# Chunk 0's state behind the turning of its outputs, and another order of tile 0's attention jobs

## What is computed

```python
for t in range(S):
    y[:, :, t] = np.einsum('bhd,bhde->bhe', q[:, :, t], state)
    v_old = np.einsum('bhde,bhd->bhe', state, k_n[:, :, t])
    state = state + beta_t * np.einsum('bhd,bhe->bhde', k_n[:, :, t], v[:, :, t] - v_old)
```

## Time and profile before

| | us |
|---|---|
| median of 3 runs | 997.12 |
| lowest, highest | 996.5, 997.6 |
| the profiled execution's own time | 997.04 |
| its span in the trace | 994.6 |
| PE busy | 953.7 |
| VectorE busy | 734.0 |
| ScalarE busy | 517.8 |
| GpSimd busy | 333.1 |

### The profile page before, as it was taken

How to read it: one execution, slowest core, us unless ns; L and a number is a source line. 1 busy time by engine, 2 the same in 40 slices (tenths; PEclk the granted TensorE clock), 3 DMA queues, 4 the chain that set the end, 5 groups by cost and what they waited for, 6 DMA issues and landing times.

```text
span 994.6 us, 23444 instructions
## 1 busy us (share of the span) xinstructions
PE 953.7 (96%) x9960; PEld 794.5 (80%) x9960; DVE 734.0 (74%) x1132; ACT 517.8 (52%) x854; POOL 333.1 (33%) x417
## 2 busy tenths in 40 slices
PE   3579999999999999999999999999999999999998
PEld 3578878888888888888788888888888888888897
DVE  5977886778687777856746668768778778687775
ACT  5664744563655456444645545545555455554543
POOL 2089748804940791296002793100101001001000
PEclk9669999999999999999999999999999999999999
DMA  9314113102200310111006311000102001010011
GB/s 213 64 36 95 33 51 66 49 17 46 64 9 19 66 49 2 24 29 48 17 4 222 96 32 64 1 1 24 41 1 65 1 11 54 0 31 3 1 33 32
DMA packets 110679, 42.50 MB, mean 43 GB/s; under 512 B 89040, under 2 KB 105936, under 8 KB 110576
## 3 DMA queue, kind: packets, MB, share of 16 engines
q1 hardware_dynamic: 105984, 39.73, 16.1%
q10 hardware_dynamic: 4592, 1.28, 0.7%
HBM read 31.56 MB, written 9.44 MB: 41 GB/s over the span
## 4 chain that ended last, share of the span: by engine, by line
PE 80%; DVE 10%; POOL 5%; issue 2%; ACT 1%; DMA 1%; ACTq 0%; DVEq 0%; POOLq 0%
PE quad L1865 15%; PE bank L1843 8%; PE bank L1844 8%; PE bank L1845 8%; PE quad L1872 8%; PE bank L1865 7%; PE quad L1843 4%; PE quad L1845 4%; PE quad L1844 4%; PE bank L1872 3%; POOL inv L566 3%; DVE blk L1037 2%; POOL blk L563 2%; PE quad L1863 1%; DVE inv L1138 1%
## 5 line engine op out<-in xcount | busy, mean ns | idle before, releaser
L1364 DVE TENSOR_TENSOR g_lo<-tmp,g_hi 128x512 fp32r<-128x512 f32 x192 | 155.4, 810 | 6.6
L1843 PE MATMUL bank<-x_hi,wi_hi 128*128 128x512 f32 x372 | 146.6, 394 | 1.3 <-issue 1.3
L1844 PE MATMUL bank<-x_lo,wi_hi 128*128 128x512 f32 x372 | 145.0, 390 | 0.0
L1845 PE MATMUL bank<-x_hi,wi_lo 128*128 128x512 f32 x372 | 145.0, 390 | 0.0
L1865 PE MATMUL quad<-g_hi,wo_hi 128*128 128x512 f32 x368 | 143.6, 390 | 0.0
L1865 PE MATMUL quad<-g_hi,wo_lo 128*128 128x512 f32 x368 | 143.4, 390 | 0.0
L566 POOL TENSOR_TENSOR inv<-inv,blk 128x31 f32<-128x31 f32 (+15 forms) x155 | 120.2, 776 | 12.1
L1872 PE MATMUL quad<-g_lo,wo_hi 128*128 128x512 f32 x368 | 117.3, 389 | 0.0
L603 POOL TENSOR_TENSOR x_lo<-x_raw,x_hi 128x1536 fp32r<-128x1536 f32 x6 | 23.2, 3859 | 269.2 <-ACT x_hi L635 269.2
L1362 DVE CAST g_hi<-tmp 128x512 fp32r<-128x512 f32 x192 | 98.0, 511 | 20.2 <-PE quad L1872 0.5
L929 ACT ACTIVATE tmp<-bank,consts 128x512 f32<-128x512 f32 x72 | 49.7, 690 | 119.0 <-PE bank L1845 119.0
(11 more groups left out here) (220 smaller groups left out, 1940.5 us busy)
## 6 DMA issues: line engine op xcount, KB each, us to landing
stage<-in_moe_w_in SPq DMA_DIRECT2D x32, 192.0 KB, 3.2
stage<-in_moe_w_out SPq DMA_DIRECT2D x8, 768.0 KB, 5.1
qn<-in_q SPq DMA_DIRECT2D x24, 192.0 KB
x_t<-x_res SPq DMA_DIRECT2D x6, 768.0 KB, 3.4
x_raw<-x_t SPq DMA_DIRECT2D x6, 768.0 KB, 5.0
res_v<-in_v SPq DMA_DIRECT2D x22, 192.0 KB, 3.7
out_x<-res SPq DMA_DIRECT2D x160, 24.0 KB, 1.5
kn<-in_k SPq DMA_DIRECT2D x32, 96.0 KB, 3.1
```

Of the source, the lines that this page charges most:

```text
L1364: nc.vector.tensor_tensor(lo, g, hi.bitcast(FP32), ALU.subtract).then_inc(g_ready, 1)
L1843: mm(dst, wi_hi[:, ft, kt, :], hi[:, kt, :], start=(kt == 0), stop=False)
L1844: mm(dst, wi_hi[:, ft, kt, :], lo[:, kt, :], start=False, stop=False)
L1845: last = mm(dst, wi_lo[:, ft, kt, :], hi[:, kt, :], start=False, stop=(kt == KT - 1))
```

## The change

`first_state()` moves on PE from the first slot of tile 0 to the end of `first()`, right behind `turn_late()` and ahead of product1(0). On VectorE `low_weights(1)` moves behind the two that make the low halves of x. In tile 0, PE's jobs T0 (of chunk 2), M1, F1, V0 and SN0 take other slots, and S0 of chunk 2 goes behind KS1. ScalarE's and VectorE's calls for them move along; on VectorE the turnings and the scaling of the inverse go to slots 11 to 13 from 9 and 11, and the four `take_blocks(2, g)` to slots 21 and 23 from 19, 20 and 21. V0 gets a lent bank and SN0 loses one. No computation is added or removed.

```diff
-ORDER_1 = ("Q0", "KS0", "P0", "T1", "S1", "T0", "M1", "F1", "V0", "SN0", "S0", "KS1", "Y0", "V1", "Q1", "SN1", "P1",
+ORDER_1 = ("Q0", "KS0", "P0", "T1", "S1", "T0", "M1", "F1", "V0", "SN0", "KS1", "S0", "Y0", "V1", "Q1", "SN1", "P1",
...
-LENT_1 = {"KS0": 4}
+LENT_1 = {"KS0": 4, "V0": 18, "KS1": 20, "V1": 22, "SN1": 24, "Y1": 26}
...
@@ ScalarE, attention_1
             take_transposes(2, "T1", knT[:, fill_of(2, 1)])
             yield
             yield
+            take_transposes(2, "T0", knT[:, fill_of(2, 0)])
+            yield
+            yield
             high_weights(5)
             yield
             yield
-            take_transposes(2, "T0", knT[:, fill_of(2, 0)])
             yield
             yield
             fill_diagonal(1, 1)
+            yield
             fill_diagonal(1, 0)
-            yield
-            yield
             yield
             take_outer(1, 0)
...
@@ VectorE, first
             low_weights(0)
-            low_weights(1)
             take_x(0, 0, "YT0")
             take_late_x()
+            low_weights(1)
             low_weights(2)
...
@@ VectorE, attention_1
             take_s(2, 1, "S1")
             yield
+            yield
+            yield
             turn_solved(1)
+            yield
             scale_inverse(1)
             yield
-            yield
             turn_inverse(1)
             yield
-            yield
             take_inner(1, 0)
+            yield
             take_inner(1, 1)
             yield
             yield
-            yield
             take_last_outer(1)
             yield
             take_delta(1, 0, "V0")
             yield
             take_state(1, 0, "SN0")
             yield
+            take_rest(1, 1, "KS1")
             take_s(2, 0, "S0")
+            yield
             take_blocks(2, 0)
             take_blocks(2, 1)
             yield
-            take_rest(1, 1, "KS1")
+            take_delta(1, 1, "V1")
+            yield
             take_blocks(2, 2)
-            yield
             take_blocks(2, 3)
-            yield
-            take_delta(1, 1, "V1")
-            yield
             yield
             take_state(1, 1, "SN1")
...
@@ PE, first and attention_1
             turn_late()
+            first_state()
 
         def attention_1():
 
-            first_state()
             yield
...
             gram(2, 1)
             yield
-            yield
-            yield
             keys_transposed(2, 0)
             yield
+            yield
+            yield
+            yield
+            yield
             merge_inner(1, (0, 1))
             yield
             yield
             yield
-            yield
             merge_outer(1, (0, 1))
             yield
             solve_values(1, 0, "V0")
             yield
             add_to_state(1, 0, "SN0")
+            yield
+            keys_on_state(1, 1, "KS1")
             gram(2, 0)
-            yield
-            yield
-            keys_on_state(1, 1, "KS1")
             yield
             read_out(1, 0, "Y0")
```

More of the change, by code:

```diff
@@ L89 @@
             place_contents(_c, _job)
[L90 to L93, removed]
+            lent = LENT_1 if _c == 1 else LENT
+            if _job in lent:
+                lend(_c, _job, lent[_job])
         elif _c + 1 < NCH:
@@ L1233, in attention_1 @@
             yield
+            take_inner(1, 0)
             yield
-            take_inner(1, 0)
             take_inner(1, 1)
-            yield
             yield
@@ L1249, in attention_1 @@
             yield
-            take_rest(1, 1, "KS1")
-            take_blocks(2, 2)
-            yield
-            take_blocks(2, 3)
-            yield
             take_delta(1, 1, "V1")
             yield
+            take_blocks(2, 2)
+            take_blocks(2, 3)
             yield
@@ L1712, in attention_1 @@
             yield
+            keys_transposed(2, 0)
             yield
             yield
-            keys_transposed(2, 0)
+            yield
+            yield
             yield
             merge_inner(1, (0, 1))
-            yield
             yield
@@ L1726, in attention_1 @@
             add_to_state(1, 0, "SN0")
-            gram(2, 0)
-            yield
             yield
             keys_on_state(1, 1, "KS1")
+            gram(2, 0)
             yield
```

## The result

The changed kernel took 1009.86 us (median of 4 runs, 1008.79 to 1011.59) where the kernel before took 997.36 us beside it: a ratio of 1.0126, 95% interval 1.0108 to 1.0144. It is slower by 12.5 us, and the forecast was 7 us. The profiled execution took 1010.21 us with a span of 1007.8 us; that of before took 997.04 with 994.6, so the two traces differ by 13.2 us, and that is the sum to be explained.

A forecast was written before the change was run, and what follows sets the result against it. The prediction took TensorE as the bound (busy 953.7 of 994.6 us). Lead at step 12, late solve and half clock, -1.0 + 6.3 + 1.7 = 7.0 us on 997.04, gave 1004.0 us (range 1001.0 to 1007.0), chance 0.58.

The forecast's parts named there:

- the front: Start of tile 0: state's matmuls fill PE's idle 1.93 us, clock stays at 2.4 GHz, product 2 of step 0 gains 2.2 us.
- s: How far PE is ahead at product 1 of step 12, tile 0: 2.2 - 1.2 = 1.0 us, bounds -0.3 and 2.9.
- clock falls at the front after all: Rival, start of tile 0: half clock despite the filled gap, product 2 of step 0 at 81.8, total 1005.6 us; chance 0.18.
- stop of 1.33 us: PE's wait near 137 us, no releaser: half kept, 0.7 us goes; if a late instruction block, wholly there again.
- 208.05 - s: Tile 1: forecast start of product 2 of step 21, which started at 201.75 before; 5.3 us later.
- late solve: GpSimd's solve of chunk 2 starts later, behind V1 and main(12), takes 49.1 us; costs 6.3 - s in tile 1.
- about even: Tile 0: new waits behind GpSimd's solve of chunk 1, less waits that go, lose 1.2 us net.
- hidden: Rival, tile 1: solve of chunk 2 takes 43 us or less, so its late start costs nothing; 996.0 us; chance 0.06.
- cancelled: Rival: solve of 46 us, 2.9 us lead and no clock price give 997.3 us, no change; chance 0.04.
- The clock behind the wait: Tile 1, after PE's 6.3 us standstill: matmuls run at half clock for a while, costing 1.7 us.
- no price in tile 1: Rival: full clock is granted soon after PE's wait in tile 1, total 1002.3 us; chance 0.14.
- PE is full, before as after: Behind 208 us: PE has no new waits, later chunks' slack is unchanged, nothing is gained or lost.

The follow-up runs named there:

- after_quiet: Changed kernel, with SyncE's load of weight piece 3 and what it issues after held back until the state's matmuls are done: 1005.25 us, ratio 1.0076.
- rest_only: Changed kernel with its front put back as before, so only the new order of tile 0's jobs is left: 1005.59 us, ratio 1.0078.
- blocks_late: Kernel before, with only the turning of blocks 2 and 3 of chunk 2 moved behind V1 and main(12) on VectorE: 1005.48 us, ratio 1.0078.
- front_split: Kernel before, low_weights(1) behind the low halves of x, half the state's matmuls at the front, half in tile 0's first slot: 997.18 us, ratio 0.9999.
- after_blocks_early: Changed kernel with all four blocks of chunk 2 turned earlier on VectorE, before V1: 1003.34 us, ratio 1.0055.
- after_quiet_early: Changed kernel with the load of weight piece 3 held back and the four blocks of chunk 2 turned earlier: 1000.39 us, ratio 1.0024.
- front_only: Kernel before with the front part of the change alone (state's matmuls and low_weights(1) moved), tile 0's order as before: 1000.49 us, ratio 1.0027.
- front_quiet: Kernel before with the front part of the change and the load of weight piece 3 held back: 997.47 us, ratio 1.0002.

## Why the prediction was wrong in size and right in kind

**The step that failed: the front.** The prediction put the moved state into 1.93 us of idle time and priced it by its own busy time, "2.01 us", so that PE "will have no idle time at all" from 72 to 74.6. The matmuls did start there, behind the turning of y_late. But 29 of 128 came 3.64 us later, the clock fell, and out(0) was 3.3 us late instead of 2.2 early. At in(12), behind which the rest of the sum is set up, the miss is 4.6 us (s = -3.62 for 1.0), and holding the load back gave 4.6 us of the time back (after_quiet). The rival "clock falls at the front after all" had the clock right and still priced out(0) at 81.8, because it too took the state as one unbroken run. The prediction even knew the mechanism: it named the instruction queue as a possible cause of the stop of 1.33 us, and did not ask the same of 128 small instructions moved into 2 us in which the DMA share was 0.86 and then 1.30. At its old place the state did not stop, because the packet was there in time. In the trace of before, 76.2 to 76.3 us:

```profile
q8 instruction: 1, 0.02, 85.9%
```

That packet ends at 77.6, and the state's first matmul came at 80.38.

**The rest of the sum held.** Set up on s, how far TensorE is ahead at in(12), the formula "208.05 - s" for out(21) can be held against four kernels:

| kernel | in(12) | s | 208.05 - s | out(21) measured |
|---|---|---|---|---|
| changed kernel | 148.22 | -3.62 | 211.67 | 211.45 |
| rest_only | 143.42 | 1.18 | 206.87 | 206.64 |
| after_quiet | 143.70 | 0.90 | 207.15 | 206.91 |
| blocks_late | 144.96 | -0.36 | 208.41 | 208.02 |

It is 0.2 to 0.4 us high each time. So the late solve was right in place, mechanism and size. Only s was not: it was forecast 1.0 and came as -3.62.

**Tile 0, "about even": right in size, by luck in part.** The 1.2 us lost from out(0) to in(12) was worked out for a TensorE that comes early. In rest_only, which does, it is 82.39 - 79.96 = 2.43 at out(0) and 1.18 at in(12), 1.25 lost. Its waits were 0.79, 1.56 and 0.28 us where 0.5, 1.65 and 0.4 had been put. But the stop of 1.33 us, of which the prediction kept half, is in none of the five kernels with the new order. The other losses must then have been 0.7 us larger than it put them, and the two errors cancel. In the changed kernel, which comes late to the solve of chunk 1, the loss is 3.62 - 3.31 = 0.3. The prediction had the fixed end of solve 1 in its sum. What it did not say is how little of a gain ahead of it can come through: in the old order, nothing of front_split's 2.34 us.

**GpSimd's solve** took 49.33 us (158.95 to 208.28) where 49.1 had been put, with VectorE idle 7.76 us at its end. The rival "hidden", which needed 43 us or less, is out, and so is "cancelled". By this case's rows VectorE's idle time is worth little here: 49.33 us with it, 49.61 without it in the kernel before.

**The clock behind the wait: right, a little small.** TensorE waited 5.89 us, and out(21) then took 4.20 us (211.45 to 215.65) against 2.21 before (201.75 to 203.96). The price is in(23)'s lateness less out(21)'s, 11.78 - 9.70 = 2.08 us, forecast 1.7. In rest_only, after_quiet and blocks_late it is 2.61, 2.15 and 1.55 us. In after_blocks_early, where the wait was 1.14 us, the clock read 1.00. The rival "no price in tile 1" is out.

**Not forecast: a stop of 1.19 us** at 232.76, without releaser, ahead of out(24). Such stops stand at the same matmuls in rest_only (0.63), blocks_late (1.12) and after_quiet_early (0.51). It stands behind 56 of 64 small matmuls each time. The prediction's "PE is full, before as after" behind 208 us is wrong by that much.

The sum of the changed kernel's trace, then: 3.62 (late at in(12)) + 6.08 (late solve, 9.70 - 3.62) + 2.08 (clock) + 1.39 (1.19 of it the last stop) = 13.17 us, against the forecast's -1.0 + 6.3 + 1.7 = 7.0. Of the 6.2 us between them the front has 4.6 (3.62 + 1.0), the last stop 1.4, the clock 0.4, and the solve -0.2. The forecast's sign was taken for nine cases in ten and its mechanism for 0.58. Of its markers, the ones on the front (clock 1.00 from 72 to 82, out(0) near 80) failed, and the ones on tile 1 came true, some 5 us late (fourth block at 158.9 for 154, end of the solve at 208.3 for 203).

**What stays open.** The stops without releaser near 137 us (0.84 to 1.99 us, in the kernels with the old order) and near 223 to 233 us (0.51 to 1.19 us) have the same sign as the one that was taken apart: in all nine of them TensorE goes on 1.2 to 1.5 us after the end of a packet of q8. (In the changed kernel that packet lies at 229.9 to 231.2, and TensorE goes on at 232.76.) The prediction's sentence by the rule of late blocks would so be right in the cause of the 1.33 us, and wrong in that it "would be there again whole". What makes those packets late is open: at 230 us no load runs, and no kernel was made to move one. Open, too, is what fills the 1.2 to 1.5 us between a packet's end and the next matmul.

## What to carry to other kernels

A gap on an engine is worth the slack of what comes next with a fixed end: follow the moved time to the next wait that ends by another engine's clock (here the solve of chunk 1) before putting it in the sum, and for every job that is pushed back, ask which long job on another engine starts from it, even one that is only awaited 50 us later. The price of a block of small instructions in a new place is not only its busy time: here TensorE ran out of instructions in it, for longer when a load ran beside it, and splitting the block or moving the load showed it. Look at where the packets of the instruction queue fall. A wait of 5 to 6 us cost twice here, once as the wait and once as the slower clock behind it.

## What the runs showed of the hardware that was not expected

TensorE stopped without a releaser within a run of 128 small matmuls, behind the 99th. With a load beside it the stop was 3.36 to 3.64 us (changed kernel, front_only, after_blocks_early), where the load's queue alone had a share of 1.13 to 1.23 between 73 and 75 us. With the load held back it was 0.90 to 1.17 us (after_quiet, front_quiet, after_quiet_early). With half the run it was gone (front_split), beside a DMA share of 1.09 in 72 to 74 us. The load moved the start of the instruction packet from 0.2 to 2.5 us behind the first matmul, and TensorE went on 1.3 to 1.5 us after its end.

The granted clock does not follow from the length of one wait alone. Half clock (1.2 GHz) came with waits of 5.3 to 5.9 us in every kernel that had them, and stayed through about 4 us of matmuls; waits of 1.1 us left it at 2.4 GHz. In between both were seen. It fell behind 1.93 us in the kernel before and behind 1.99 us in front_quiet (near 137 us). It stayed behind 1.66 us at the first of these places in rest_only, and behind 1.72 us at the second in blocks_late.
